# Splitting the first two merged operands straight from PSUM on VectorE, and a new order of three ScalarE copies and exponentials

## The reference

```python
p_packed = sm_attn(p, k, v)              # 32 packed rows per head attend to 576 keys
out = sm_attn(q, p_packed, p_packed)     # 576 queries attend to the 32 packed rows
x = out.transpose(0, 2, 1, 3).reshape(4608, 512)
h = x @ w_in                             # 512 -> 1024
solu = h * softmax(h)
x = layer_norm(solu) * g_ln @ w_out      # 1024 -> 512
h = maximum(x @ w1, x @ w2, x @ w3)      # 512 -> 768
out = h @ w_out2                         # 768 -> 512
```

## Time and profile before

| | us |
|---|---|
| median of three runs | 1042.54 |
| lowest and highest | 1041.39, 1042.71 |
| the profiled execution's own time | 1041.39 |
| its span | 1039.6 |
| TensorE busy | 1002.4 (96%) |
| VectorE busy | 602.6 (58%) |
| ScalarE busy | 348.4 (34%) |
| GpSimd busy | 267.7 (26%) |

### The profile page before, as it was taken

How to read it: one execution, slowest core, us unless ns; L and a number is a source line. 1 busy time by engine, 2 the same in 40 slices (tenths; PEclk the granted TensorE clock), 3 DMA queues, 4 the chain that set the end, 5 groups by cost and what they waited for, 6 DMA issues and landing times.

```text
span 1039.6 us, 14971 instructions
## 1 busy us (share of the span) xinstructions
PE 1002.4 (96%) x6050; PEld 808.1 (78%) x6050; DVE 602.6 (58%) x984; ACT 348.4 (34%) x559; POOL 267.7 (26%) x228
## 2 busy tenths in 40 slices
PE   7988788999999999999999999999999999999998
PEld 5655457878888888888888888888888888888887
DVE  2888877757557577556365635556256735553021
ACT  4766633433423324325122332114222331223111
POOL 0377662866958396510000000000000000000000
PEclk9999989999999999999999999999999999999999
DMA  8988724254643364115745535543455444542341
GB/s 286 383 298 276 281 96 168 77 189 151 236 165 112 136 224 163 74 47 223 291 166 191 180 125 212 187 174 142 164 204 203 152 160 167 190 152 92 112 162 41
DMA packets 47269, 183.17 MB, mean 176 GB/s; under 512 B 8160, under 2 KB 8160, under 8 KB 37600
## 3 DMA queue, kind: packets, MB, share of 16 engines
q1 hardware_dynamic: 40976, 147.21, 39.8%
q0 software_dynamic: 6224, 35.00, 9.0%
HBM read 134.62 MB, written 47.58 MB: 175 GB/s over the span
## 4 chain that ended last, share of the span: by engine, by line
PE 80%; DVE 11%; ACT 3%; issue 3%; POOL 2%; DMA 0%; ACTq 0%; POOLq 0%
PE ps L1123 28%; PE ps L760 25%; PE ps L1155 14%; PE ps L1146 5%; PE ps L1024 2%; PE ps L866 1%; DVE h_lo L1513 1%; DVE spot L1811 1%; ACT a L1227 1%; DVE packedT L1571 1%; DVE spot L1802 1%; DVE a2T L1606 1%; DVE bn L1698 1%; PE ps L774 1%; PE ps L847 1%
## 5 line engine op out<-in xcount | busy, mean ns | idle before, releaser
L1123 PE MATMUL ps<-ys,slot 128*128 128x512 f32 x1512 | 345.8, 390 | 0.5
L1123 PEld LDWEIGHTS ps<-ys,slot 128*128 128x128 f32 x1512 | 283.3, 188 | 62.4 <-ACT spot L1198 3.9
L1802 DVE TENSOR_TENSOR spot<-ps,spot 128x512 f32<-128x512 f32 x108 | 74.3, 688 | 104.3 <-PE ps L1123 75.1
L1198 ACT ACTIVATE spot<-ps 128x512 f32<-128x512 f32 x90 | 52.8, 595 | 207.7 <-PE ps L1123 196.6
L760 PE MATMUL ps<-ln_hi,w_out_s_lo 128*128 128x512 f32 x280 | 109.0, 389 | 0.0
L760 PE MATMUL ps<-ln_lo,w_out_s_hi 128*128 128x512 f32 x280 | 109.0, 389 | 0.0
L760 PE MATMUL ps<-ln_hi,w_out_s_hi 128*128 128x512 f32 x280 | 109.0, 389 | 0.0
L1155 PE MATMUL ps<-w_out_s_lo,h_hi 128*128 128x512 f32 x216 | 84.1, 389 | 0.0
L1155 PE MATMUL ps<-w_out_s_hi,h_hi 128*128 128x512 f32 x216 | 84.1, 389 | 0.0
L1155 PE MATMUL ps<-w_out_s_hi,h_lo 128*128 128x512 f32 x216 | 84.1, 389 | 0.0
L1329 ACT ACTIVATE u<-ps,neg_max 128x1024 f32<-128x1024 f32 x36 | 40.2, 1117 | 123.9 <-DVE neg_max L1680 123.9
(11 more groups left out here) (158 smaller groups left out, 1479.8 us busy)
## 6 DMA issues: line engine op xcount, KB each, us to landing
slot<-w_operands SPq DMA_DIRECT2D x36, 1792.0 KB, 7.2
w_operands<-stage POOLq DMA_DIRECT2D x18, 1024.0 KB, 4.9
v_raw<-in_v_dram SPq DMA_DIRECT2D x8, 1152.0 KB, 5.9
q_raw<-in_q_dram SPq DMA_DIRECT2D x32, 288.0 KB, 5.2
y_features<-yst SPq DMA_DIRECT2D x9, 1024.0 KB, 4.4
y_raw<-y_features SPq DMA_DIRECT2D x9, 1024.0 KB, 5.3
out_dram<-spot SPq DMA_DIRECT2D x36, 256.0 KB, 2.1
slot<-w_operands SPq DMA_DIRECT2D x9, 1024.0 KB, 5.1
```

The costliest lines, as they stand in the source:

```text
L1123: last = pe.matmul(ps[:, group_bank(g, k), :], w[:, a - 1, i, kk, :], ys[:, b, j, kk, :], start=n < 4 and kk == 0 and e == 0, stop=kk == K ...
L1198: return act.activation(dst, src, ACT.Copy)
L1802: dve.tensor_tensor(dst[:, :], a, b, op).then_inc(ready, 1)
```

## The change

- `copy_m` of batches 0 and 1 writes M out of PSUM straight into the hi part of `m_s[b]`. The tensors `merged_first` are gone.
- `split_merged` is gone from GpSimd. VectorE makes both lo parts in the same step as the merge, from PSUM and hi, two subtractions of 128x1024 in each of steps 0 and 1. One stands ahead of `copy_q`, one behind it, both ahead of `max1`. The `lo_m` of steps 2 and 3 are gone.
- TensorE's `scores1(b, g)` for b = 2 and 3, which overwrites the banks of M, also waits for `lo_m(b-2, g)`.
- ScalarE runs `exp1(b+2, 0)` at the end of step b rather than as `exp1(b+1, 0)` near the start of the next step. So it comes ahead of that step's first two k copies.
- ScalarE's `copy_q(b+1, 1)` comes behind `exp2(b, 1)` rather than ahead of it.

```diff
-    m_hi, m_low = sem("m_hi"), [sem(f"m_low{g}") for g in range(QUADS)]
-    a_hi, a_low = sem("a_hi"), sem("a_low")
+    m_low, a_hi, a_low = sem("m_low"), sem("a_hi"), sem("a_low")
...
     def merged_of(b):
-        if b < 2:
-            return merged_first[b]
         return merged_last if b == B - 1 else merged
...
-            def split_merged(b):
-
-                hi, low = (m_s[b][:, e, :, :] for e in range(2))
-                raw = merged_of(b)
-                for g in range(QUADS):
-                    pool.wait_ge(m_copied[g], b + 1)
-                    if b == 1:
-
-                        pool.wait_ge(m_hi, QUADS)
-                        for low_ready in m_low:
-                            pool.wait_ge(low_ready, 1)
-                    pool.tensor_scalar(hi[:, g, :], raw[:, g, :], 1.0, None, ALU.mult).then_inc(m_hi, 1)
-                    if g == 0:
-                        pool.wait_ge(m_hi, QUADS * b + 1)
-                        pool.tensor_tensor(low[:, g, :], raw[:, g, :], hi[:, g, :].bitcast(F32), ALU.subtract)\
-                            .then_inc(m_low[g], 1)
...
-                if 0 < b < 3:
-                    split_merged(b - 1)
...
                     pe.wait_ge(m_copied[g], b - 1)
+                    if b < 4:
+                        pe.wait_ge(m_low, QUADS * (b - 2) + g + 1)
...
                 if batch < 2:
-                    for low_ready in m_low:
-                        pe.wait_ge(low_ready, batch + 1)
+                    pe.wait_ge(m_low, QUADS * (batch + 1))
                     pe.wait_ge(a_low, batch + 1)
...
-                dst = merged_of(b)[:, g, :]
+                dst = m_s[b][:, 0, g, :] if b < 2 else merged_of(b)[:, g, :]
...
                 if second:
-                    exp1(b + 1, 0)
                     exp1(b + 1, 1)
...
                     copy_q(b + 1, 0)
-                    copy_q(b + 1, 1)
                 if third:
                     exp2(b, 1)
                 if second:
+                    copy_q(b + 1, 1)
                     copy_q(b + 1, 2)
...
+                if first:
+                    exp1(b + 2, 0)
...
-            def lo_m(b):
-
-                g = QUADS - 1
-                dve.wait_ge(m_hi, QUADS * b + QUADS)
-                hi, low = (m_s[b][:, e, g, :] for e in range(2))
-                lo(low, merged_of(b)[:, g, :], hi).then_inc(m_low[g], 1)
+            def lo_m(b, g):
+                dve.wait_ge(m_copied[g], b + 1)
+                hi, low = (m_s[b][:, e, g, :].rearrange("r (n c) -> r n c", n=WIDE) for e in range(2))
+                lo(low, ps[:, wide_banks[g]:wide_banks[g] + WIDE, :], hi).then_inc(m_low, 1)
...
+                if direct:
+                    lo_m(b, 0)
                 if second:
                     copy_q(b + 1, QH)
-                if third and 1 < b < 4:
-                    lo_m(b - 2)
+                if direct:
+                    lo_m(b, 1)
```

More of the change, by code:

```diff
@@ L178, in packed_attention_ffn @@
     a2T = place_at(yst_base, "a2T", [P, QUADS, S])
-    merged_first = (place_at(odd_base, "merged_first0", [P, QUADS, FF1]),
-                    place_at(yst_base - 2 * 1024 * 4, "merged_first1", [P, QUADS, FF1]))
     slot_shape = [P, 7, 2, KH, P]
```

## The result

| | before | after |
|---|---|---|
| median, us | 1041.97 | 1051.47 |
| lowest and highest | 1041.39, 1042.71 | 1048.66, 1053.2 |
| ratio, 95% interval | | 1.0087 [1.0069, 1.0103] |
| profiled execution, its span | 1041.39, 1039.6 | 1052.93, 1051.1 |

The change made the kernel slower by 9 us where 3.3 were forecast. The sign was right, the size was not, and the time lies outside the range. The profiled execution of after is one of its slower ones; the traces differ by 11.5 us in span, the medians by 9.5.

What follows compares the result with a forecast made beforehand. TensorE, busy 96% of the span, bounds the kernel; in the attention it waits for copies, maxima and exponentials. Terms 2.75+2.75-0.71+0.81-1.42-0.65-0.34+0.10 sum to +3.3 us, 1045.9 against the median 1042.54; range 1042.4 to 1049.0.

Steps and rivals of the forecast that it cites:

- part (c): TensorE's scores1 in steps 0 and 1 waiting for lo_m: costs nothing, 0.3 us each as the upper end.
- its own sign of being wrong: A half-clock stretch of TensorE near 45 or 60 us would show the forecast wrong.
- part (b): ScalarE's exp1(b+2,0) ahead of two k copies: with the subtractions, +2.75 us in each of steps 0 and 1.
- The rival: TensorE's clock: waits in steps 0 and 1 each draw a half-clock stretch, +2.6 us in all, 1048.5; chance 0.07.
- (a): Two VectorE subtractions ahead of max1 in steps 0 and 1 delay the negated maximum by 2.26 us.
- The lower end, 1.80: Cost in each of steps 0 and 1 with ScalarE's old order, the k copies being done during the wait.
- First step: The exponential slips in ahead of the k copies while ScalarE idles, so the second starts earlier: -0.71 us.
- Step 4: At its end the k copies no longer run in the wait for the maximum: +0.81 us.
- (d): GpSimd's splits go away, giving back 1.42 us in step 2 and 0.65 us in step 3.
- (e): lo_m leaves steps 2 and 3: -0.34 us in step 3 (full -1.13 without the new order), nothing in step 2.
- The relief: Rival: GpSimd's relief pays for it all, 5.0 us more coming back, 1040.9 us, no visible change; chance 0.12.
- (f): copy_q(b+1,1) behind exp2(b,1) delays the merge by 0.6 us, mostly covered: +0.10 us, ends 0 and +0.6.

Runs made afterwards that it cites:

- With the waits filled: Short extra 128x256 matmuls in TensorE's waits of steps 0 and 1: on the kernel after 1.0053 of before; on it with ScalarE's old order 1.0042.
- the exponential alone: The kernel before with only the exponential exp1(b+2,0) moved ahead of the k copies: 1.0040 of before.
- with the collision removed: The kernel after with short extra matmuls in steps 0, 1 and 4 to 6, and GpSimd's w_out subtraction waiting for VectorE's reciprocal: 1.0034 of before, 1045.06 us.
- the q copy alone: The kernel before with only copy_q(b+1,1) moved behind exp2(b,1): 1.0001 of before.
- another kernel: The kernel before with the first step's exponential moved and five extra 128x256 matmuls ahead of scores2(6,0): 0.9992 of before.

## Why the prediction was wrong

**What failed** is part (c), the wait of TensorE for the subtractions, which was priced at nothing, "0.3 each as the upper end". It asked only how late the second maximum would be, and left out what the wait does to TensorE's clock; the clock stood only among the rivals, at 1.3 us for a stretch and 7 in 100. Measured, the waits of steps 0 and 1 draw stretches of 6.8 us at 41.8 and 62.3 us, where the prediction had put its own sign of being wrong, and the transposes and scores behind the wait are themselves the path. With the waits filled, 2.1 to 2.2 us come back in step 0 and 1.4 in step 1. In step 1 it would be 2.3 without the unexplained stop, which is worked out and not shown. The clock takes some 0.8 more in step 5 and 1.4 behind the last a1. There TensorE waits 1.71 us at a time for the k copies of part (b) in steps 4 and 5, 3.32 with that part alone; which wait draws the late stretches of the kernel after isn't settled. The rival had the right mechanism; its number was taken from a stretch half as long, and half of that stretch's 2.91 busy us is 1.46 rather than 1.3.

**(a), (b), the subtractions and the order.** Right in mechanism, and right in size once the clock is whole: 2.77 in step 0 against 2.75, and 3.69 in step 1, where the stop is. The lower end, 1.80 with the old order, was wrong: 3.6 and 3.4 were measured with the waits filled, because the k transposes queue behind the second scores.

**First step.** 1.0 in the profile, 0.71 forecast. One execution doesn't settle it: in the twelve profiles with this exponential moved, the transposes of a1 that begin step 0 start at 28.4 to 29.6 us, against 29.9 to 30.0 in the four without it.

**Step 4.** The +0.81 is there and the collision behind it is not in the prediction: it looked for what GpSimd's splits had delayed and not for what a shifted addition would run into. Together +1.65, and 0.88 with the collision removed (17.23).

**Step 5** was forecast at nothing, measured +1.53, clock and collision; 0.11 with both removed.

**(d), (e).** Right: step 3 17.09, as forecast to the digit; step 2 18.66 against 18.46. From a1's transposes to packed's both take 6.00 us, 6.05 forecast. Without the new order step 3 took 16.3 us, which is the "full -1.13" of part (e). The relief did not pay for all, by far.

**(f).** Right: nothing that shows in the whole, though step by step it moves 0.4 to 0.5 us.

**PSUM as a source.** The subtraction took 1.23 and 1.22 us from PSUM in after, and 1.215 from SBUF in before. The Trainium skill, "VectorE: DVE Perf Modes", section on the TRN2 errata, gives 120 cycles for a PSUM source and 58 for SBUF, an estimated 65 ns more. The traces do not show it: the difference is 0.01 to 0.02 us.

## What to carry to other kernels

A wait put on TensorE in a stage where its own work is the path can cost more than its length: ask what stands behind it, and whether it leaves the engine without work in one piece (here the clock fell after 2.35 us of it). Moving work of ScalarE or VectorE only because that engine idles can empty TensorE by the same stroke. A few useless matmuls in a wait, no longer than the wait, are a cheap test of it, and here a gain.

## What the runs showed of the hardware

TensorE fell to half clock in a wait of 2.35 us (kernel after), in one of 2.37 (the q copy alone) and in one of 3.32 (the exponential alone). In the kernel before, a wait of 2.67 us at 98 us drew none in the profile shown and one of 6.8 us in another kernel whose steps were the same up to there. Executions of one program differ in this, and the time goes with it: before ran from 1040.1 us at a mean granted TensorE clock of 0.996 to 1045.2 at 0.992, the kernel after from 1048.7 at 0.995 to 1053.2 at 0.987.

A VectorE addition on two columns can take 1.92 us: it ended with GpSimd's 128x1024 subtraction (107.17 and 107.15 us), and took 0.17 once GpSimd was made to wait for it. The Trainium skill, "SBUF — State Buffer", section on the two separate sides, calls the port pair that the two engines share "an exclusive lock, not a bandwidth split", whose loser waits for the whole instruction. It says so for VectorE operations in a mode that uses both ports or with two SBUF inputs. This trace agrees in the wait; in which mode the addition ran it doesn't show.
